# Routing 18 of 24 token tiles inside attention, a shorter chain for the last six, and gates from a second set of products

## The chip, the cores and the metric

One of the eight cores of a Trainium2 chip runs the program. The metric is the device time of one execution in microseconds (us). Its engines are TensorE (PE, with its weight loads as PEld), VectorE (DVE), ScalarE (ACT), GpSimd (POOL) and SyncE (SP), which here only issues DMAs.

## What is computed

```
q, k, v: (4, 8, 768, 64)       # attention with 4 sink keys and a window of 128
scores = where(is_sink | in_window, scale * q @ k.T, -1e9)
a = softmax(scores);  x = (a @ v) as rows: (3072, 512)

logits = x @ w_gate + modality_bias[modality_id]          # 8 experts
e = argmax(logits);   gate = softmax(logits)[e]
y[rows of e] = gate * (relu(x[rows of e] @ w1[e]) @ w2[e])   # w1: 512x1024

h = y @ w_in;  out = (h * sigmoid(1.702 h)) @ w_out       # w_in: 512x2048
```

## The kernel before

Attention runs over 4 batches of 48 steps each (8 heads, 6 query tiles of 128 rows, `each_step`). In step n PE multiplies the scores of tile n (`scores`), turns the probabilities of tile n - 3 (`turn_probs`, copied out of PSUM by ACT, and by DVE for the last tile of a head: `move_probs`) and weighs the values of tile n - 4 (`weigh_values`). DVE masks each tile (`mask_scores`), and every sixth step it scales a finished head (`finish_head`), which also gives that head's share of the router logits. Heads go out to `x_rows` in DRAM in pairs (`store_pair`). GpSimd only splits q and k of coming heads into a high and a low part (`split_qk`); it is through with the last head at 206.6 us.

Each product of large matrices is three products of such high and low parts (`fp32r`).

Behind attention comes the routing, for all 24 tiles of 128 tokens at once. DVE adds the biases, takes the maximum, makes a one-hot of the chosen expert (ties go to the lowest number), and the gate from `exp` on ACT. PE multiplies the one-hot with a triangle and with ones (L738, L739), DVE sums the tile counts by doubling (L1244), and so knows each token's place among the tokens of its expert. From counts it makes `table` (which expert each of 32 slots of 128 rows belongs to, where a run of one expert begins, how many there are), signals `runs_ready`, and SP loads the first expert's weights in four quarters of 1 MB (`load_run`). DVE then makes masks: `oh_val` (tile of the slot times token number, gate high, gate low) and `oh_slot` (row in the slot). The inverse, which token stands in which row of which slot, is the sum of 24 products of these (L744). From it come `gather_i`, `scatter_i` and `gates`.

The experts run slot by slot: POOL gathers the 128 rows (`gather`), PE turns them (`turn_xs`), ACT and DVE split them (`xs_high`, `xs_low`), PE multiplies up (`up`), turns h (`turn_h`), multiplies down (`down`), DVE scales by the gate and POOL scatters. For slot 0 `up` needs the first split and the high and low parts of w1 (`w_highs` on ACT, `w_lows` on DVE). The loads of the next expert (`load_run` in a loop) wait until the low parts of the same quarter are made. This data uses 3 experts in 26 slots. Then the dense layers follow.

Every order is written by hand: each engine executes its list in order, and semaphores are all that connects them. The helper `then` makes an engine wait for its own last instruction.

## Time and profile before

| what | value |
| --- | --- |
| median of 3 runs (lowest to highest) | 1146.12 us (1145.73 to 1149.06) |
| the profiled execution | 1148.82 us |
| its span in the profile | 1146.6 us |
| PE busy | 1103.9 us, 96% |
| DVE, ACT, POOL busy | 37%, 33%, 26% |
| chain that ended last | PE 92%, DVE 4% |
| attention | 0 to 231 us |
| routing, until the first expert product | 231 to 272 us |
| experts, then dense layers | 272 us to the end |

Busy time is that of instructions on the engine. In a timeline a row starts with its start and its length in us; at its end, in brackets, stands how long the engine had been idle and who ended that. Matmuls are pipelined, so their lengths overlap, and distances of starts say more. `PEclk` is the granted clock of PE, 1.00 at 2.4 GHz and 0.50 at 1.2 GHz.

### The profile page before, as it was taken

To read this page: it belongs to the slowest core of one execution; us is meant where nothing else is said; L and a number is where in the kernel's file an instruction comes from. 1 tells how busy PE (TensorE), PEld (TensorE's weight loads), DVE (VectorE), ACT (ScalarE), POOL (GpSimd) and SP (SyncE) were. 2 spreads that over 40 slices of the span, in tenths; PEclk is the share of its full clock that TensorE was granted. 3 is DMA by queue.
4 is the path that set the end of the run, shared out by engine and by line. 5 is a ranking of instruction groups with operands and counts; after the bars stand their busy time and mean duration, and the time that the engine had idled before them with its cause. 6 is when DMAs were issued, how large, how long until landed. Compare 5 with 4: busy or idle time off the path is not lost.

```text
span 1146.6 us, 18452 instructions
## 1 busy us (share of the span) xinstructions
PE 1103.9 (96%) x5844; PEld 933.2 (81%) x5845; DVE 429.7 (37%) x1109; ACT 376.8 (33%) x780; POOL 299.9 (26%) x394
## 2 busy tenths in 40 slices
PE   9999999926999999999999999999999999999998
PEld 9999999915888888888887888888888888888887
DVE  5666656685222224222265223323223222222222
ACT  3666666613222233212254222222222222222222
POOL 8888889202662212212110001001001001000100
PEclk9999999956999999999999999999999999999999
DMA  9999998136111115211133001101000100000000
GB/s 221 229 247 238 234 239 224 47 102 242 37 37 55 37 46 192 67 53 46 37 107 123 19 1 46 27 0 46 18 9 37 27 9 19 18 0 0 37 1 37
DMA packets 57390, 92.01 MB, mean 80 GB/s; under 512 B 7936, under 2 KB 32768, under 8 KB 57344
## 3 DMA queue, kind: packets, MB, share of 16 engines
q1 hardware_dynamic: 51584, 72.56, 23.7%
q0 software_dynamic: 5760, 18.89, 4.8%
q8 instruction: 23, 0.38, 0.2%
q14 instruction: 23, 0.19, 0.1%
HBM read 72.02 MB, written 19.41 MB: 80 GB/s over the span
## 4 chain that ended last, share of the span: by engine, by line
PE 92%; DVE 4%; issue 1%; ACT 1%; POOL 1%; DVEq 0%; ACTq 0%; POOLq 0%
PE psum L837 8%; PE psum L828 8%; PE psum L830 8%; PE psum L839 8%; PE psum L829 8%; PE psum L838 8%; PE psum L686 6%; PE psum L770 4%; PE psum L771 4%; PE psum L772 4%; PE psum L795 4%; PE psum L797 4%; PE psum L796 4%; PE psum L661 3%; PE psum L649 2%; PE psum L782 2%
## 5 line engine op out<-in xcount | busy, mean ns | idle before, releaser
L1421 DVE TENSOR_TENSOR g<-psum,g 128x512 f32<-128x512 f32 x96 | 66.3, 691 | 306.5 <-ACT g L1024 306.4
L1024 ACT ACTIVATE g<-psum 128x512 f32<-128x512 f32 x96 | 57.5, 599 | 319.0 <-PE psum L830 316.1
L828 PE MATMUL psum<-x2T,win_hi 128*128 (+1 forms) x384 | 153.1, 399 | 2.3 <-DVE g L1421 2.3
L837 PE MATMUL psum<-w_hi,gT_hi 128*128 128x512 f32 x384 | 153.2, 399 | 0.0
L830 PE MATMUL psum<-x2T,win_lo 128*128 (+1 forms) x384 | 152.5, 397 | 0.0
L829 PE MATMUL psum<-x2T,win_hi 128*128 (+1 forms) x384 | 152.0, 396 | 0.0
L839 PE MATMUL psum<-w_hi,gT_lo 128*128 128x512 f32 x384 | 150.4, 392 | 0.0
L838 PE MATMUL psum<-w_lo,gT_hi 128*128 128x512 f32 x384 | 149.3, 389 | 0.0
L618 POOL DMA_INDIRECT out<-o_out,out_rows x20 | 19.5, 976 | 424.3 <-ACT o_out L1037 419.7
L686 PE MATMUL psum<-v_sb,pT 128*128 128x73 f32 x704 | 106.0, 269 | 1.7
L1148 DVE CUSTOM_DVE_ANT_0 s_msk<-psum,mask_sb 128x260 f32<-128x260 f32 (+1 forms) x192 | 74.8, 403 | 74.1 <-PE psum L650 38.9
L686 PEld LDWEIGHTS psum<-v_sb,pT 128*128 128x128 f32 x704 | 93.4, 191 | 8.2 <-DVE pT L1160 6.7
L908 ACT ACTIVATE probs<-s_msk,negmax 128x260 f32<-128x260 f32 (+1 forms) x192 | 93.4, 495 | 12.3 <-DVE negmax L1148 12.3
L1424 DVE TENSOR_TENSOR gT_lo<-g,gT_hi 128x512 fp32r<-128x512 f32 x96 | 66.5, 693 | 65.9 <-ACT gT_hi L1028 65.9
L770 PE MATMUL psum<-w_hi,xsT_hi 128*128 128x512 f32 x208 | 84.5, 406 | 4.1 <-DVE xsT_lo L1375 4.1
L828 PEld LDWEIGHTS psum<-x2T,win_hi 128*128 128x128 f32 x384 | 72.5, 189 | 19.2 <-issue 2.7
L830 PEld LDWEIGHTS psum<-x2T,win_lo 128*128 128x128 f32 x384 | 72.4, 189 | 18.1
L829 PEld LDWEIGHTS psum<-x2T,win_hi 128*128 128x128 f32 x384 | 72.4, 188 | 17.1
L839 PEld LDWEIGHTS psum<-w_hi,gT_lo 128*128 128x128 f32 x384 | 72.0, 188 | 17.2
L838 PEld LDWEIGHTS psum<-w_lo,gT_hi 128*128 128x128 f32 x384 | 72.2, 188 | 15.7
L1028 ACT CAST gT_hi<-g 128x512 fp32r<-128x512 f32 x96 | 59.6, 620 | 75.7 <-DVE g L1421 75.7
L837 PEld LDWEIGHTS psum<-w_hi,gT_hi 128*128 128x128 f32 x384 | 72.1, 188 | 14.8
(200 smaller groups left out, 1950.7 us busy)
## 6 DMA issues: line engine op xcount, KB each, us to landing
qk_raw<-qkT SPq DMA_DIRECT2D x64, 384.0 KB, 9.2
stage<-w SPq DMA_DIRECT2D x12, 1024.0 KB, 6.1
x<-y_rows SPq DMA_DIRECT2D x24, 256.5 KB, 2.6
vT_sb<-vT SPq DMA_DIRECT2D x16, 384.0 KB, 10.4
v_sb<-vP SPq DMA_DIRECT2D x16, 384.0 KB
x_rows<-x_sb SPq DMA_DIRECT2D x16, 384.0 KB, 8.0
win_raw<-w_in SPq DMA_DIRECT2D x16, 256.0 KB, 10.3
stage<-w_out SPq DMA_DIRECT2D x4, 1024.0 KB, 6.5
```

The costliest lines, as they stand in the source:

```text
L686: mm = pe.matmul(o, pT[:, n % 2, k * P:(k + 1) * P], v_sb[:, c, kb, half * VEXT:(half + 1) * VEXT], start=(i == 0 and k == 0), stop=(k == ...
L770: pe.matmul(psum[:, HB[hf], :], xsT_hi[:, c, :], hi, start=(c == 0), stop=False)
L828: pe.matmul(bank, wh, hi, start=(c == 0), stop=False)
L829: pe.matmul(bank, wh, lo, start=False, stop=False)
L830: mm = pe.matmul(bank, win_lo[:, c, f * P:(f + 1) * P], hi, start=False, stop=(c == CH - 1))
L837: pe.matmul(psum[:, OB[t], :], gh, hi, start=(f == 0), stop=False)
L838: pe.matmul(psum[:, OB[t], :], gh, lo, start=False, stop=False)
L839: return pe.matmul(psum[:, OB[t], :], gT_lo[:, f % 4, t * P:(t + 1) * P], hi, start=False, stop=(f == F2C - 1))
L908: act.activation(probs[:, n % RING, 0:width[i]], s_msk[:, n % RING, 0:width[i]], ACT.Exp, bias=negmax[:, n % 8:n % 8 + 1], scale=-1.0).the ...
L1148: dve.tensor_tensor_reduce(s_msk[:, n % RING, 0:width[i]], psum[:, S_ps[n % 3], 0:width[i]], mask_sb[:, min(i, MASKS - 1), 0:width[i]], -S ...
L1421: dve.tensor_tensor(g32[:, f % 2, :], psum[:, FB[f % 2], :], g32[:, f % 2, :], ALU.mult)\
L1424: dve.tensor_tensor(gT_lo[:, f % 4, :], g32[:, f % 2, :], gT_hi[:, f % 4, :].bitcast(F32), ALU.subtract).then_inc(gT_split, 1)
```

## The change

Bias, maximum, one-hot, exponential and gate of the first 18 tiles (batches 0 to 2) move into steps 29 to 43 of the last batch, on DVE, with the exponential on ACT at step 39. POOL adds up their one-hots tile by tile (`seen`), PE multiplies their ranks at step 41 (`rank_early`), and POOL makes their `oh_slot`. For the six tiles of the last batch seven heads are summed at step 49, and behind the last head DVE has a short list (`add_last_head` to `choose`). Their ranks come from eight small products, with counts over all tiles among them, so the sum by doubling is gone. `x_sb` of the last head is scaled only behind the one-hot.

The first expert's number is computed ahead of the tables and has a semaphore of its own, `expert_known`; SP loads its w1 then, its w2 once the first gather has landed, and reads the table later. The inverse is multiplied for the token numbers alone; `gather_i` comes from it in one operation, and the gates come from a second set of 24 products. The tables (`make_tables`, `make_spare`) move behind the second low part of w1 on DVE, and the end of the scatter table goes to POOL, between its second and third gather. Between these products PE gets dummy products of the identity: 16, 40, 12 and 8 (`keep_going`).

```diff
@@ SP
+            sp.wait_ge(expert_known, 1)
+            load_run(0, sp.value_load(first_e[0:1, 0:1], min_val=0, max_val=E - 1))
+            load_win(B * PAIRS - 1)
             sp.wait_ge(runs_ready, 1)
...
-            load_run(0, sp.value_load(table[0:1, RUN_E:RUN_E + 1], min_val=0, max_val=E - 1))
@@ SP, load_run, quarter q of run 0
+                        if q == 2:
+                            sp.wait_ge(gathered, 16)
@@ POOL
+            pool.wait_ge(onehot_ready, 1)
+            for t in range(PRE):
+                then(pool.tensor_tensor(seen[:, t + 1, :], seen[:, t, :].bitcast(F32), onehot[:, t, :].bitcast(F32),
+                                        ALU.add))
+            pool.sem_inc(tiles_seen, 1)
+
+            pool.wait_ge(rows_known, 1)
+            for t in range(PRE):
+                pool.tensor_scalar(oh_slot[:, t, :], iota_row[:], rank_p[:, t:t + 1], None, ALU.is_equal)\
+                    .then_inc(rows_marked, 1)
+
+            def finish_scatter():
...
+                pool.wait_ge(spare_known, 1)
+                then(pool.tensor_tensor(t1, iota_slot[:], t1, ALU.subtract))
...
+                then(pool.tensor_scalar(scatter_i[:, 0:SLOTS], t1, iota_dump[:, 0:1], None, ALU.add))
...
+            gather(0)
+            gather(1)
+            finish_scatter()
+            gather(2)
+            pool.wait_ge(runs_ready, 1)
             total = pool.value_load(table[0:1, TOTAL:TOTAL + 1], min_val=NTILE - 4, max_val=SLOTS - 4) + 4
-            for t in range(3):
-                gather(t)
-            pool.wait_ge(tables_ready, 2)
@@ PE
+            def rank_early():
+
+                pe.wait_ge(onehot_ready, 1)
+                pe.wait_ge(tiles_seen, 1)
...
+                pe.matmul(at, tri[:], onehot[:, 0:PRE, :].rearrange("p t e -> p (t e)"), start=True, stop=False)
+                pe.matmul(at, ones[:], seen[:, 0:PRE, :].rearrange("p t e -> p (t e)"), start=False, stop=True)\
+                    .then_inc(ranks_ready, 1)
...
+            def keep_going(times):
+                for _ in range(times):
+                    pe.matmul(psum[:, XB, 0:P], ident[:], ident[:], start=True, stop=True)
+
+            pe.wait_ge(scores_masked, B * HT + AHEAD)
+            keep_going(16)
+
+            pe.wait_ge(onehot_ready, 2)
...
+            mm.then_inc(ranks_ready, 1)
+            keep_going(40)
+
+            pe.wait_ge(rows_marked, PRE)
             for t in range(NTILE):
-                if t % GT == 0:
-                    pe.wait_ge(ohs_ready, t // GT + 1)
-                mm = pe.matmul(psum[:, 2, 0:3 * SLOTS], oh_slot[:, t, :], oh_val[:, t].rearrange("p a s -> p (a s)"),
+                if t in (0, PRE):
+                    pe.wait_ge(ohs_ready, 1 + t // PRE)
+                mm = pe.matmul(psum[:, 2, 0:SLOTS], oh_slot[:, t, :], tile_tok[:, t, :],
                                start=(t == 0), stop=(t == NTILE - 1))
...
+            keep_going(12)
+
+            pe.wait_ge(heads_done, B * H + AHEAD)
+            pe.wait_ge(gates_marked, 1)
+            for t in range(NTILE):
+                mm = pe.matmul(psum[:, O_ps[1], 0:2 * SLOTS], oh_slot[:, t, :],
+                               tile_gate[:, t].rearrange("p a s -> p (a s)"), start=(t == 0), stop=(t == NTILE - 1))
+            mm.then_inc(gates_ready, 1)
+            keep_going(8)
...
+            turn_xs(0)
+            up(0, 0)
+            turn_xs(1)
+            pe.wait_ge(runs_ready, 1)
@@ ACT
+            first_high(0, w1_high)
             xs_high(0)
+            first_high(1, w1_high)
+            first_high(2, w2_high)
+            first_high(3, w2_high)
             relu(0)
             xs_high(1)
@@ DVE, the last batch
+            def route_early(n):
+
+                if n == 29:
+                    then(dve.tensor_scalar(from_end[:], iota_row[:, 0:E], -1.0, float(E), ALU.mult, ALU.add))
+                    pick_bias(0)
+                if n == 30:
+                    for m in range(1, NM):
+                        pick_bias(m)
+                if n == 31:
+                    add_biases(pre)
+                    find_best(pre)
+                if n == 33:
+                    find_lead(pre)
+                if n == 35:
+                    then(dve.tensor_scalar(seen[:, 0, :], from_end[:], 0.0, None, ALU.mult))
+                    choose(pre)
...
+                if n == 41:
+                    make_gates(pre, 1)
+                if n == 42:
+                    take_ranks(pre, psum[:, VW_ps, 0:PRE * E].rearrange("p (t e) -> p t e", e=E), 1)
...
@@ DVE, behind attention
+            add_last_head()
+            find_best(own)
+            find_lead(own)
+            choose(own)
...
+            dve.tensor_scalar(first_e[:], e_cnt[:, 1, 0:1], -1.0, float(E), ALU.mult, ALU.add).then_inc(expert_known, 1)
...
+            first_low(0, w1_high, w1_split)
             xs_low(0)
+            first_low(1, w1_high, w1_split)
+            make_slot_gates()
+            make_tables()
+            make_spare()
...
+            first_low(2, w2_high, w2_split)
             xs_low(1)
+            first_low(3, w2_high, w2_split)
```

Three places show how the lists stand. PE first, from attention's last product to the first product of an expert; `ident` alone is a dummy, `ident,xs` turns the first slot's rows, `w_hi,xsT_hi` is the expert's. Before:

```order
L691 MATMUL psum<-v_sinks,pT_sinks 128x4x73
L738 MATMUL psum<-onehot,tri 128x192
L739 MATMUL psum<-onehot,ones 128x192
L744 MATMUL psum<-oh_val,oh_slot 128x96 x24
L800 TENSOR_LOAD table
L800 ISA x2
L755 MATMUL psum<-ident,xs 128x128 x4
```

PE in the changed kernel, from the 16 dummies on (seven more small products of one-hots stand between the ranks' first and the 40):

```order
L825 MATMUL psum<-onehot,ones 128x16
L825 MATMUL psum<-onehot,ones 128x8
L809 MATMUL psum<-ident 128x128 x40
L835 MATMUL psum<-tile_tok,oh_slot 128x32 x24
L809 MATMUL psum<-ident 128x128 x12
L843 MATMUL psum<-tile_gate,oh_slot 128x64 x24
L809 MATMUL psum<-ident 128x128 x8
L854 MATMUL psum<-ident,xs 128x128 x4
```

Two sets of products and 76 dummies now stand ahead of the first rows, and the read of the table is gone from there.

DVE in steps 30 to 32 of the last batch; `s_msk` is a tile's mask, `pT` the copy that PE waits for. Before:

```order
L1148 ISA s_msk,negmax<-psum,mask_sb 128x128
L1148 ISA negmax 128x1
L1148 ISA s_msk,negmax<-psum,mask_sb 128x260
L1148 ISA negmax 128x1
L1148 ISA s_msk,negmax<-psum,mask_sb 128x260
L1148 ISA negmax 128x1
L1159 COPY pT_sinks<-psum 128x128
L1160 COPY pT<-psum 128x256
```

DVE there in the changed kernel (four more operations, up to `bias_of`, stand ahead of the first row's mask, in step 29):

```order
L1245 TENSOR_SCALAR mod_eq<-mod_f 128x24
L1247 TENSOR_TENSOR biases<-mod_eq,bias_sb 128x192
L1249 TENSOR_TENSOR bias_of<-bias_of,biases 128x192
L1354 ISA s_msk,negmax<-psum,mask_sb 128x260
L1354 ISA negmax 128x1
L1259 TENSOR_TENSOR lg<-lg,bias_of 128x144
L1268 TENSOR_REDUCE best<-lg 128x18
L1354 ISA s_msk,negmax<-psum,mask_sb 128x260
L1354 ISA negmax 128x1
L1365 COPY pT_sinks<-psum 128x128
L1366 COPY pT<-psum 128x256
```

Nine operations now stand between the masks ahead of the copy.

POOL from the last split of q and k to the third gather; brackets name what a row waits for. Before:

```order
L549 TENSOR_TENSOR q_st<-qk_raw,q_st 64x768 [waits qk_rounded]
L552 TENSOR_TENSOR k_lo<-qk_raw,k_hi 128x6x128 [waits qk_split]
L554 TENSOR_TENSOR k_lo<-qk_raw,k_hi 128x6x4
L592 TENSOR_LOAD table [waits x_stored3,x_stored2,tables_ready,x_stored1,x_stored0]
L592 ISA x2
L574 COPY gather_col<-gather_i 128x1
L578 DMA xs<-x_rows,gather_col 128x512 [waits gather_set,xs_turned]
```

POOL in the changed kernel, where seven more rows of the same kind stand between the two on `tokens` and the last:

```order
L591 TENSOR_TENSOR seen<-seen,onehot 128x8 [waits onehot_ready]
L591 TENSOR_TENSOR seen<-seen,onehot 128x8 [waits pool_step] x17
L597 TENSOR_SCALAR oh_slot<-iota_row,rank_p 128x128 [waits pool_step,rows_known]
L597 TENSOR_SCALAR oh_slot<-iota_row,rank_p 128x128 x17
L635 DMA xs<-x_rows,gather_i 128x512 [waits tables_ready,x_stored3,xs_turned,x_stored2,x_stored0,x_stored1]
L635 DMA xs<-x_rows,gather_i 128x512 [waits xs_turned]
L604 TENSOR_TENSOR tokens<-iota_slot,tokens 128x32 [waits spare_known]
L605 TENSOR_TENSOR tokens<-tokens 128x32 [waits pool_step]
```

The first gather stands without a table read or copy ahead of it, the third behind nine operations.

## Rows read from the trace of the kernel before

**Rows 1.** Windows: stretch, length, busy PE, PEld, DVE, ACT, POOL, clock, DMA, GB/s.

```profile
231.00:272.00 41.00, 8.41 (x33) 7.37 (x34) 34.06 (x100) 10.04 (x8) 5.26 (x4) 0.53 0.41 138
```

**Rows 2.** Timeline behind attention's last product, DVE.

```profile
231.03 0.17 DVE L1165 TENSOR_SCALAR rden<-psum 128x6 f32<-128x6 f32 x1 [1.30 <-PE psum L691]
231.23 0.19 DVE L1167 RECIPROCAL rden<-rden 128x6 f32<-128x6 f32 x1
```

**Rows 3.** Timeline from the table to the inverse products, all engines.

```profile
247.13 0.20 DVE L1287 CAST table<-table_f 128x75 int32<-128x75 f32 x1
...
250.48 25.98 SPq L428 DMA_DIRECT2D stage<-w  x8
250.49 0.96 DVE L1310 TENSOR_TENSOR tile_eq<-iota_row,pos_t 128x768 f32<-128x768 f32 x1
...
255.20 5.36 PE L744 MATMUL psum<-oh_val,oh_slot 128*128 128x96 f32 x24 [17.82 <-DVE oh_slot L1316]
255.63 1.90 ACT L965 CAST w_hi<-stage 128x2048 fp32r<-128x2048 f32 x1 [5.96 <-DMA stage<-w]
```

**Rows 4.** Timeline from the first gather to the first expert product, all engines.

```profile
263.55 1.15 POOL L578 DMA_INDIRECT xs<-x_rows,gather_col  x1 [0.96 <-POOL gather_col L574]
...
266.37 4.49 DVE L1360 TENSOR_TENSOR w_lo<-stage,w_hi 128x2048 fp32r<-128x2048 f32 x2 [0.95 <-DVE gates L1346]
...
267.12 1.12 PE L755 MATMUL psum<-ident,xs 128*128 128x128 f32 x4 [6.57 <-DMA xs<-x_rows,gather_col]
...
268.28 0.59 ACT L981 CAST xsT_hi<-psum 128x512 fp32r<-128x512 f32 x1 [2.66 <-PE psum L755]
...
271.71 0.77 PE L770 MATMUL psum<-w_hi,xsT_hi 128*128 128x512 f32 x1 [3.48 <-DVE xsT_lo L1375]
```

**Rows 5.** Timelines of SP, POOL, DVE and PE, second gather to first down projection.

```profile
268.89 7.57 SPq L428 DMA_DIRECT2D stage<-w  x4
...
269.54 2.17 POOL L578 DMA_INDIRECT xs<-x_rows,gather_col  x1 [0.83 <-POOL gather_col L574]
276.63 0.18 POOL L574 COPY gather_col<-gather_i 128x1 int32<-128x1 int32 x1 [4.92 <-DMA xs<-x_rows,gather_col]
...
281.47 0.69 DVE L1375 TENSOR_TENSOR xsT_lo<-psum,xsT_hi 128x512 fp32r<-128x512 f32 x1 [5.61 <-ACT xsT_hi L981]
...
287.99 0.60 PE L755 MATMUL psum<-ident,xs 128*128 128x128 f32 x4
288.34 0.48 PE L795 MATMUL psum<-w_hi,hT_hi 128*128 128x512 f32 x1
```

**Rows 6.** Windows where the clock falls and where it rises again (PEclk is third last).

```profile
233.60:233.80 0.20, 0.00 (x0) 0.00 (x0) 0.17 (x2) 0.00 (x0) 0.00 (x0) 0.50 0.95 289
...
277.00:278.00 1.00, 1.00 (x4) 0.81 (x3) 0.00 (x0) 0.60 (x1) 0.00 (x0) 0.54 1.06 391
```

**Rows 7.** Windows of L728, the identity products at the start (PE, PEld, PEclk, DMA, GB/s).

```profile
13.30:14.25 0.95, 0.89 (x8) 0.92 (x8) 1.00 0.97 207
```

**Rows 8.** Timelines of DVE and PE, steps 31 to 36 of the last batch.

```profile
209.03 0.43 DVE L1148 CUSTOM_DVE_ANT_0 s_msk<-psum,mask_sb 128x260 f32<-128x260 f32 x1 [0.50 <-ACT probs L908]
...
209.94 0.43 DVE L1148 CUSTOM_DVE_ANT_0 s_msk<-psum,mask_sb 128x260 f32<-128x260 f32 x1 [0.47 <-PE psum L650]
...
210.29 0.29 DVE L1159 COPY pT_sinks<-psum 128x128 f32<-128x128 f32 x1
...
210.96 0.67 PE L686 MATMUL psum<-v_sb,pT 128*128 128x73 f32 x4
...
214.97 0.36 DVE L1137 TENSOR_TENSOR bias_of<-c,bias_sb 128x192 f32<-128x192 f32 x1
```

**Rows 9.** POOL: timeline of two dependent operations, then one line's durations.

```profile
6.20 0.29 POOL L500 TENSOR_SCALAR_AFFINE_SELECT mask_sb<-mask_sb 128x128 f32<-128x128 f32 x1
6.63 0.29 POOL L502 TENSOR_SCALAR_AFFINE_SELECT mask_sb<-mask_sb 128x128 f32<-128x128 f32 x1
...
L554 POOL TENSOR_TENSOR k_lo<-qk_raw,k_hi x31: 218/228/237, 16.0 to 206.3; 128x24 fp32r<-128x24 f32 x31
```

More of the change, by code:

```diff
@@ L221, in program @@
         e_cnt = place("e_cnt", [P, 6, E])
-        tokens = place("tokens", [P, 3, SLOTS])
+        tokens = place("tokens", [P, 4, SLOTS])
         table_f = place("table_f", [P, TAB])
@@ L943, in step, with gate_exps @@
                     spread_sinks(b, n // (2 * QT))
-            each_step(step)
-            act.wait_ge(shifted, 1)
-            act.activation(r_b, r_a, ACT.Exp).then_inc(exped, 1)
-            act.wait_ge(runs_ready, 1)
-            for c in range(PAIRS):
-                act.wait_ge(x_stored[c], DMA * B + DMA)
-            last = act.value_load(table[0:1, TOTAL:TOTAL + 1], min_val=NTILE - 4, max_val=SLOTS - 4) + 2
+                if b == B - 1 and n == EXP_AT:
+                    gate_exps(slice(0, PRE), 1)
+            def gate_exps(tiles, part):
+                act.wait_ge(shifted, part)
+                act.activation(exps_of[:, tiles, :], below[:, tiles, :], ACT.Exp).then_inc(exped, 1)
+            each_step(step)
+            gate_exps(slice(PRE, NTILE), 2)
             def run_and_first(t):
@@ new lines, in _, with col, row, shape_of @@
+            e_col = iota_row[:, 0:E].rearrange("p (s o) -> p s o", o=1).broadcast_to(sq)
+            e_row = iota_row[:, 0:E].rearrange("p (o e) -> p o e", o=1).broadcast_to(sq)
+            full, pre, own = [P, NTILE, E], slice(0, PRE), slice(PRE, NTILE)
+            def col(v, shape):
+                return v.rearrange("p (t o) -> p t o", o=1).broadcast_to(shape)
+            def row(v, shape):
+                return v.rearrange("p (o e) -> p o e", o=1).broadcast_to(shape)
+            def shape_of(tiles):
+                return [P, tiles.stop - tiles.start, E]
@@ new lines, in _ @@
+            busy, runs_before = e_cnt[:, 4, :], e_cnt[:, 5, :]
+            then(dve.tensor_tensor(tend, base_e[:], tiles, ALU.add))
+            then(dve.tensor_scalar(busy, tiles, 0.0, None, ALU.is_gt))
+            tab = [P, SLOTS, E]
+            ends, counted = (e_tab[:, k].rearrange("p (s e) -> p s e", e=E) for k in range(2))
+            slot_col = col(iota_row[:, 0:SLOTS], tab)
+            then(dve.tensor_tensor(ends, slot_col, e_cnt[:, 3:4, :].broadcast_to(tab), ALU.is_ge))
+            then(dve.tensor_tensor(counted, ends, e_cnt[:, 4:5, :].broadcast_to(tab), ALU.mult))
```

427 lines of the change are left out of this document (242 added, 185 removed).

## The prediction

> **What bounds the kernel now.** I read the windows first, then the timeline from 226 to 300 us, then the timelines of DVE, PE and POOL inside the last batch. PE is busy almost everywhere except between the two halves of the program: from 231 to 272 us it works 8.4 of 41 us and its clock is down to 0.53 on average [rows 1]. Attention's last product is done at 231.0 (DVE, which waited for it, starts at 231.03 [rows 2]); the first expert matmul starts at 271.71 [rows 4]. In between one thing at a time happens: DVE computes logits, one-hots and ranks, all tables, four wide masks; PE multiplies 24 tiles; then the row indices, the gather, a transpose, a split. From 288.34 on, where the first down projection starts [rows 5], PE has no wait that the change reaches, so I carry the change from 231.0 to that point: what it wins there is the gain. The profiled execution took 1148.82 us with a span of 1146.6, so 2.2 us lie outside it, and the median of the runs is 1146.12. I take the gain off the median.
>
> **Step 1, routing inside attention (a loss).** DVE gets bias, maximum and one-hot work of the first 18 tiles in steps 29 to 36 of the last batch. A narrow DVE operation costs 0.20 us start to start [rows 2], one of 192 columns 0.40 (0.36 and the hand-over) [rows 8], so one of 144 some 0.31. Step 29: three narrow and one wide, 1.0. Step 30: one narrow, two wide, 1.0. Step 31: two of 144, 0.6. That is 2.6 us ahead of the copy of the turned probabilities of step 29, in a stretch where DVE idles 0.50 and 0.47 [rows 8]. PE takes that copy at once: copies start at 210.29, last 0.6, and the product that reads them starts at 210.96 [rows 8]. So PE loses 2.6 - 1.0 = **1.6 us**. The biases that this replaces stood at step 36, with slack behind them; there the new work (about 1.6 us) only takes their place. At steps 41 to 43 DVE gets 2.0 us more, but PE's own delay (next) covers it.
>
> The one-hot of the early tiles is then ready near 216.6 (before's step 35 mask, plus 1.6, plus 0.5 of its own). POOL adds it up in 18 dependent additions of 8 columns. The nearest rows are a dependent pair of POOL operations, 0.43 us start to start, and its 24-column addition of 0.23 [rows 9]: bounds 0.28 and 0.43 each. I take 0.35, nearer to the small one plus the hand-over (0.14 between the rows of the pair). 18 x 0.35 = 6.3, so 222.9, and PE stands before its early rank product at 222.0: **0.9 us** (0 to 2.4), and 0.2 for the two products. Attention ends 2.7 us later, at 233.7; the bounds are 1.0 and 4.5. All times below are without this 2.7, which is taken off at the end.
>
> **Step 2, from attention to the row indices.** The last batch's chain on DVE is now eight operations of at most 48 columns behind the last product (0.20 to 0.24 each), 231.03 to about 233.1. But PE's queue has 16 dummy matmuls ahead of the rank products. A dummy is two records; 8 records take 0.89 us at full clock [rows 7], 0.22 a dummy, so 16 are 3.6: ranks start at 234.5, not 233.1. The 8 rank products go at the rate of small products, 24 in 5.36 us at half clock [rows 3], 0.11 each at full clock: 0.9, done 235.5. Then 40 dummies: 8.9, to **244.4**. DVE in that time needs six narrow operations (first expert, 236.8), two, two of 64 columns, two of 192, one narrow (238.7), the wide comparison of 768 columns at 0.96 [rows 3], the tokens (1.0), and its six tiles' rows (0.96 and a narrow one): 242.0. So it isn't DVE that is late, it is the dummies, by 2.4 us. 24 inverse products: 2.6, to 247.0. Row indices in one operation: 247.3.
>
> **Step 3, to the first expert matmul.** The gather goes straight from those indices; POOL started 0.96 us after its copy and PE had the rows 3.57 us later [rows 4], so rows are there at 251.8. That is cover, not path: PE first does 12 dummies (2.7, hidden behind DVE) and waits for the gates' masks. DVE: four narrow operations, two of 768 columns: 0.9 + 2.0, ready 250.2. 24 gate products 2.6, 8 dummies 1.8, transposes 0.60 [rows 5]: 255.2. ACT's high part 0.59 [rows 4] and DVE's low part 0.69 [rows 5], with hand-overs 1.4: **256.6**, against 271.71. Weights do not decide it: expert known at 236.8, SP issues within 1 to 3 us, the first quarter arrives 5.1 us after issue and is cast in 1.90 [rows 3], its low part takes 2.25 [rows 4]; all that ends by 252.5.
>
> **Step 4, from there to the first down projection.** ACT casts the second quarter only behind the first rows: 255.9 + 1.9 = 257.8, DVE's low part 2.25: 260.1. An up projection took 5.8 at full clock, start included (24 matmuls from the split at 281.47 + 0.69 to 287.99 [rows 5]); half of one is 2.8, so PE waits 0.7 and ends the second half at 262.9. Behind the low part DVE has slot gates (0.4), tables (15 operations, 3.4: 263.9), spare counts (1.3: 265.2), a low part (2.25) and only then the second tile's split (0.7): 268.2. The second up projection therefore starts at 268.2 and ends at 273.8; that is a wait of 2.3 us that the kernel before hasn't got.
> POOL finishes the scatter table before its third gather: spare counts at 265.2, nine operations of about 0.37: 268.5, gather starts 269.3. Alone a gather lands after 3.6. But SP has the table at 263.9, reads four registers (3.1 us from the table, 247.13 + 0.20, to the first issue at 250.48 in the kernel before [rows 3]) and issues the next expert's weights from 267 on. The gather that started at 269.54 under such loads (SP issued from 268.89 on) was back at 276.63, 7.1 us [rows 5]. With three quarters queued at 2.7 each behind the 5.1 (267.0 + 5.1 + 5.4 = 277.5) I take 8: 277.3. PE waits 3.5, transposes, starts down at **277.7**. Before: 288.34. Gain 10.6, less 2.7 of step 1: **7.9 us**. Part of it is the clock: the kernel before ran the first 6.1 us at half rate (0.50 from 233.6, up in the slice 277 to 278 [rows 6]), 3.0 us lost, which the dummies are to save.
>
> **Rivals.**
> *The third gather isn't held up.* It lands 3.6 us after it starts, at 272.9, before PE wants it: 3.5 us more, a gain of 11.4, **1134.7**. For it: the transfer is small, and how many quarters are queued at that moment depends on SP's register reads. Against it: the 7.1 us of a gather behind fresh loads [rows 5]. Chance 0.20. The Trainium skill, DMA: Bandwidth & Descriptors, section Queues, rings and completion order, says that a DMA engine takes turns between the queues that have work, packet by packet; by that rule the gather would pass the weights and the sum would be this rival's. The trace does not agree well: under loads a gather took twice its time alone.
> *The clock falls in the new waits.* PE is idle 2.3 and 3.5 us in step 4; in the kernel before it was down by 233.6, 2.6 us after the last work [rows 6]. If it falls once where nothing hides it, the price is that of the kernel before: 3.0 us. Gain 4.9, **1141.2**. Chance 0.15; against it, PE has worked densely up to the wait.
> *POOL's additions are slow.* If each costs what POOL shows between a copy and its dependent DMA, 0.83 [rows 5], 18 take 14.9 and PE stands 9.5 us instead of 0.9: gain -0.7, **1146.8**. It eats the gain from 0.8 us an addition on. Chance 0.05.
> *Slower: the dummies run at half clock.* If the half rate (1.2 GHz) has set in before the first block of them, each dummy costs 0.44, and the small products double. The first two blocks, ranks and inverse products then take 16.0 us more; the third block, 5.3, outlasts DVE's masks by 2.2; gate products, last block and transposes take 4.9 more: 23.0 in all. The gain turns into a loss of 15.2: **1161.3**. It eats the gain from some 36 half-rate dummies on, fewer if the products fall with them. Against it: the clock reads 1.00 over the stretch of the same dummies at the start [rows 7], and PE has no gap before them. Chance 0.05.
> *It does less than it says:* the dummies may cover what was won, as step 2 has it for 2.4 us; that is in the forecast.
>
> **How the numbers follow.** Forecast 0.53 at 1146.1 - 7.9 = **1138.2**, its own range 1135 to 1141 (step 1: +1.7, -1.8; POOL and register reads 1 us each). Gather early 0.20 (1132.5 to 1136.5), clock 0.15, slow additions 0.05, slow dummies 0.05, something smaller than 3.4 us for other reasons 0.02. The range from 1132.5 to 1142.5 leaves out the last three and the tails. A measurement of this kernel can tell about 0.3%, 3.4 us, from no change. Faster by more: nearly all of 0.53 and 0.20 and most of the clock's 0.15: 0.86. Within: the rest of these and the slow additions, 0.08. Slower: 0.06.
>
> **What would show it.** In the profile of the changed kernel: PE waiting at the copy of step 29 by 1.6 us and before the early rank product by about 1; its clock at 1.00 from 231 on; the inverse products starting right behind the 40 dummies and not behind a DVE wait; the first expert matmul 12 us earlier than 271.71; waits of PE on the second split (2.3) and on the third gather (3.5), with weights in flight. It is wrong if the third gather lands in under 5 us, if the early additions take above 8 us in all, or if PE waits for the inverse masks instead of running dummies.

## The result, and the profile after

The changed kernel takes 1150.32 us (median of 19 runs, 1147.94 to 1158.09), the kernel before 1146.72 beside it (19 runs, 1145.73 to 1149.06): ratio 1.0035, 95% interval [1.002, 1.005]. It is slower by 0.35%, and outside the predicted range. The profiled execution took 1149.0 us with a span of 1147.1, so it is one of the shorter ones, 0.2 us above the profiled one of before (0.5 in the spans); the medians are 3.6 us apart. The 19 executions of before lie in two groups, 1145.7 to 1146.7 and 1148.1 to 1149.1 us, and the profiled one is of the upper group. The two traces explain 0.5 us; the other 3.1 are differences between executions of one kernel that they do not show.

| stretch (us) | before | forecast | after |
| --- | --- | --- | --- |
| attention's end | 231.03 | +2.7 | 238.22 (+7.2) |
| from there to the first expert product | 40.7 | 25.6 | 26.65 |
| from there to the first down projection | 16.6 | 21.1 | 24.0 |
| first down projection starts at | 288.34 | 280.4 | 288.86 |

From there to the end it is 858.3 us before and 858.2 after. So in these traces the routing chain did get shorter by 14 us, and all of it was given back: 7.2 in attention, 7.4 between the first expert product and the first down projection.

The equal ends hide two falls of PE's clock that cancel. In both kernels PE waits 2.28 us for `g` ahead of the first product of the dense layers. Up to that product the changed kernel loses 1.5 us (318.1 us from the first down projection, 316.6 before), all of it at half clock behind 288.86. Behind it the traced execution of before loses 1.5 us, since its clock falls there and that of the changed kernel does not: the same products take 0.63 and 0.40 us. Rows of PE, before and then after:

```profile
604.93 0.49 PE L828 MATMUL psum<-x2T,win_hi 128*128 x1 [2.28 <-DVE g L1421]
...
606.24 0.63 PE L829 MATMUL psum<-x2T,win_hi 128*128 x1
```

```profile
606.96 0.49 PE L928 MATMUL psum<-x2T,win_hi 128*128 x1 [2.28 <-DVE g L1610]
...
607.74 0.40 PE L928 MATMUL psum<-x2T,win_hi 128*128 x1
```

PE's timeline after, the rows at which the forecast has a term (start, length, at the end in brackets the idle time before and who ended it). `pT` is the copy of the turned tiles 29 and 41, `tile_tok` the inverse products, `tile_gate` the gate products, `ident` alone dummies, `ident,xs` the turning of rows, `w_hi,xsT_hi` up projections, `w_hi,hT_hi` the first down projection:

```profile
215.18 0.67 PE L745 MATMUL psum<-v_sb,pT 128*128 128x73 f32 x4 [2.36 <-DVE pT L1366]
...
230.15 0.67 PE L745 MATMUL psum<-v_sb,pT 128*128 128x73 f32 x4 [1.41 <-DVE pT L1366]
...
251.34 2.83 PE L835 MATMUL psum<-tile_tok,oh_slot 128*128 128x32 f32 x24
254.01 4.55 PE L809 MATMUL psum<-ident 128*128 128x128 f32 x24
258.32 2.85 PE L843 MATMUL psum<-tile_gate,oh_slot 128*128 128x64 f32 x24
...
264.87 0.50 PE L869 MATMUL psum<-w_hi,xsT_hi 128*128 128x512 f32 x1 [1.40 <-DVE xsT_lo L1550]
268.28 0.50 PE L869 MATMUL psum<-w_hi,xsT_hi 128*128 128x512 f32 x1 [0.39 <-DVE w_lo L1570]
276.42 0.79 PE L869 MATMUL psum<-w_hi,xsT_hi 128*128 128x512 f32 x1 [2.13 <-DVE xsT_lo L1550]
287.89 0.66 PE L854 MATMUL psum<-ident,xs 128*128 128x128 f32 x4 [3.12 <-DMA xs<-x_rows,gather_i]
288.86 0.79 PE L894 MATMUL psum<-w_hi,hT_hi 128*128 128x512 f32 x1 [0.31 <-issue]
```

Windows after (columns as in [rows 1]; the clock is third last). The first answers [rows 1]: PE is busy 25.3 of 26.7 us where it was busy 8.4 of 41. The others are where the clock is down:

```profile
238.20:264.90 26.70, 25.30 (x213) 25.06 (x212) 15.70 (x46) 5.02 (x6) 3.77 (x5) 0.94 0.45 148
...
230.00:232.00 2.00, 1.85 (x9) 1.55 (x10) 0.44 (x3) 0.11 (x1) 2.00 (x4) 0.71 0.04 8
232.00:234.00 2.00, 2.00 (x11) 2.00 (x11) 1.49 (x7) 0.85 (x3) 2.00 (x5) 0.50 0.00 0
...
254.00:256.00 2.00, 2.00 (x14) 2.00 (x14) 1.59 (x6) 0.00 (x0) 0.39 (x1) 0.68 0.00 0
256.00:258.00 2.00, 2.00 (x12) 2.00 (x10) 2.00 (x3) 0.00 (x0) 1.28 (x1) 0.50 0.05 8
...
277.00:281.00 4.00, 4.00 (x11) 3.12 (x10) 2.58 (x3) 0.00 (x0) 3.35 (x7) 0.50 1.05 401
...
290.00:292.00 2.00, 2.00 (x6) 1.53 (x5) 0.00 (x0) 0.00 (x0) 1.99 (x2) 0.50 0.46 127
```

The mean clock rose from 0.979 to 0.993. What a low clock costs on the path changed less. Before, the half rate fell into 41 us in which PE had little to do; it cost 3.0 us in the first expert products and 1.5 at 605, and it doubled the 24 inverse products (5.36 us for 2.67), for which DVE stood 2.44 us (before):

```profile
260.59 0.19 DVE L1323 TENSOR_SCALAR tokens<-psum 128x32 f32<-128x32 f32 x1 [2.44 <-PE psum L744]
```

In the changed kernel it comes four times up to 293 us, each time under work, where the forecast had it at full rate. A window of 2 us at 0.50 loses 1.0. It loses 1.7 us at 230 to 235, of which 1.35 reach the end of attention; 1.6 in the dummies at 254 (24 records take 4.3 us, 2.7 at full clock), of which 1.1 are on the path, since the gate masks come late too; 2.6 in the second up projection (hidden, since the third gather is awaited anyway); 1.6 behind 288.86. That is some 4.1 us on the path.

DVE after, steps 29 to 32, ahead of PE's row at 215.18. It answers [rows 8]; the first column is the start:

```profile
210.94 0.36 DVE L1247 TENSOR_TENSOR bias_of<-mod_eq,bias_sb 128x192 f32<-128x192 f32 x1
211.53 0.29 DVE L1354 CUSTOM_DVE_ANT_0 s_msk<-psum,mask_sb 128x128 f32<-128x128 f32 x1 [0.23 <-DVE bias_of L1247]
...
213.62 0.30 DVE L1268 TENSOR_REDUCE best<-lg 128x18 f32<-128x144 f32 x1
214.15 0.43 DVE L1354 CUSTOM_DVE_ANT_0 s_msk<-psum,mask_sb 128x260 f32<-128x260 f32 x1 [0.23 <-DVE best L1268]
...
214.71 0.41 DVE L1366 COPY pT<-psum 128x256 f32<-128x256 f32 x1
```

Each group of routing work costs 0.23 us more than its operations: `then` waits for the last of them before the mask may start.

GpSimd and DVE after, where the scatter table is finished ahead of the third gather, and the line of the 18 additions:

```profile
273.30 2.28 DVE L1570 TENSOR_TENSOR w_lo<-stage,w_hi 128x2048 fp32r<-128x2048 f32 x1
273.47 2.22 POOL L604 TENSOR_TENSOR tokens<-iota_slot,tokens 128x32 f32<-128x32 f32 x1 [8.25 <-DVE tokens L1518]
...
275.50 0.68 DVE L1550 TENSOR_TENSOR xsT_lo<-psum,xsT_hi 128x512 fp32r<-128x512 f32 x1
275.77 0.25 POOL L605 TENSOR_TENSOR tokens<-tokens 128x32 f32<-128x32 f32 x1
276.10 2.28 DVE L1570 TENSOR_TENSOR w_lo<-stage,w_hi 128x2048 fp32r<-128x2048 f32 x1
276.12 2.42 POOL L606 TENSOR_SCALAR tokens<-tokens 128x32 f32<-128x32 f32 x1
...
219.23 5.12 POOL L591 TENSOR_TENSOR seen<-seen,onehot 128x8 fp32r<-128x8 f32 x18 [11.74 <-DVE onehot L1279]
```

The same kind of operation on 32 columns takes 0.25 us beside DVE's `xsT_lo`, which reads one operand from PSUM, and 2.2 to 2.4 when it meets a low part of w, which reads both from SBUF, the on-chip memory; it then ends 0.1 to 0.2 us behind that.

### The profile page after: what moved, and what is told of

It reads as the page before. It is cut to its first block, busy times and chain, and to the rows that moved or that the text cites. A ratio compares the mean times of both kernels' runs of the same rounds, so it can differ in the third digit from the quotient of the medians.

```text
span 1147.1 us, 18894 instructions
## 1 busy us (share of the span) xinstructions
PE 1124.4 (98%) x6026; PEld 953.5 (83%) x6027; DVE 426.7 (37%) x1100; ACT 378.5 (33%) x781; POOL 321.0 (28%) x436
## 4 chain that ended last, share of the span: by engine, by line
PE 90%; DVE 3%; issue 2%; ACT 2%; POOL 1%; DMA 1%; ACTq 0%; DVEq 0%; POOLq 0%
PE psum L937 8%; PE psum L928 8%; PE psum L939 8%; PE psum L930 8%; PE psum L929 8%; PE psum L938 8%; PE psum L745 5%; PE psum L894 4%; PE psum L896 4%; PE psum L895 4%; PE psum L871 4%; PE psum L870 4%; PE psum L869 4%; PE psum L720 2%; PE psum L881 2%
## 5 line engine op out<-in xcount | busy, mean ns | idle before, releaser
L894 PE MATMUL psum<-w_hi,hT_hi 128*128 128x512 f32 x208 | 84.5, 406 | 0.5 <-issue 0.3
```

The lines of the kernel that those rows point to most:

```text
L894: pe.matmul(psum[:, YB, :], hT_hi[:, f, :], hi, start=(f == 0), stop=False)
```

## The experiments

All are compared with the kernel before, run beside them on the same chip; its median there was 1148.26 (a1 to a4), 1146.85 (b1 to b4), 1148.44 (c1 to c3, a5) and 1146.76 (d1), its lowest and highest values within 0.6 us of those above. Its median still moves by 1.7 us, so differences of medians between these sets of runs are good to about 1.7 us. Each kernel of the table ran 4 to 11 times.

| kernel | median us | ratio to before, 95% interval |
| --- | --- | --- |
| a1_head_waits | 1150.34 | 1.0014 [1.0003, 1.0025] |
| a2_spread | 1149.69 | 1.0018 [1.0007, 1.0029] |
| a3_dummies | 1144.46 | 0.9960 [0.9945, 0.9976] |
| a4_order | 1143.32 | 0.9957 [0.9942, 0.9971] |
| b1_slots | 1152.89 | 1.0046 [1.0024, 1.0068] |
| b2_combo | 1137.70 | 0.9924 [0.9908, 0.9941] |
| b3_best | 1142.81 | 0.9952 [0.9927, 0.9976] |
| b4_late | 1151.57 | 1.0031 [1.0015, 1.0047] |
| c1_free | 1144.60 | 0.9976 [0.9965, 0.9987] |
| c2_all | 1133.83 | 0.9884 [0.9867, 0.9902] |
| c3_no_dummies | 1143.73 | 0.9964 [0.9947, 0.9981] |
| a5_gather_first | 1143.75 | 0.9974 [0.9962, 0.9985] |
| d1_tuned | 1128.94 | 0.9838 [0.9824, 0.9852] |

**What attention lost: own waits, or the work?** The first run takes only waits away: behind a head's logits DVE does not wait for itself.

```diff
@@ finish_head, add_heads (a1_head_waits)
-                then(part)
+                if b == B - 1 and h == H - 1: then(part)
+                else: steps[0] += 1; part.then_inc(dve_step, 1)
+                dve.wait_ge(dve_step, steps[0])        # ahead of the sum over heads
```

> The changed kernel, with DVE no longer waiting for its own last instruction behind each head's logits and behind the sum over heads of batches 0 to 2. In the changed kernel's trace the first mask behind that sum is 0.22 us late, and PE is later by 0.43 to 0.47 us at step 9 of every batch, 1.8 us in all by step 28 of the last batch. Theory A (the added waits are the cause): scores of step 28 of the last batch start at 205.7 to 206.1 us instead of 207.64, the span shrinks by 1.5 to 1.9 us. Theory B (the shift comes from somewhere else, such as the fetch of a longer instruction list): it stays within 0.4 us of 207.64.

The start of the scores of step 28 of the last batch, against before (205.68), is +1.96 in the changed kernel and +0.7 here: the waits cost 1.3 us, less than theory A's 1.5 to 1.9 and far more than theory B's 0.4. The median does not show it (1150.34 for 1150.32, from two sets of runs). But the rest shows what a wait of PE can trigger. Row of PE and window of a1_head_waits:

```profile
213.87 1.13 PE L745 MATMUL psum<-v_sb,pT 128*128 128x73 f32 x4 [2.34 <-DVE pT L1370]
```

```profile
214.00:230.00 16.00, 16.00 (x71) 15.40 (x72) 6.45 (x33) 4.71 (x14) 3.67 (x18) 0.50 0.00 0
```

The same wait of 2.3 us at the copy of tile 29 as in the changed kernel, and behind it 16 us of attention at half clock, with PE busy all along. This execution took 1156.67 us; the changed kernel has three of its length (1158), which were not traced. So this wait costs 2.2 us in one trace and 10 in another.

The second run keeps that edit and moves the early routing:

```diff
@@ route_early (a2_spread): steps
-  29, 30, 31, 33, 35, 36, 37, 41, 42, 43
+  1, 9, 13, 21, 25, 33, 45, and the gates of the early tiles behind attention
```

> As the run before it, and the early tiles' routing is cut into pieces that stand where DVE idled 1.1 us or more in the kernel before (steps 1, 9, 13, 21, 25, 33, 45 of the last batch) instead of steps 29 to 43; the early gates' sum goes behind the last head. Theory A (DVE's queue ahead of the copies of steps 29 and 41 is what holds PE up, and the clock falls in the waits it makes): attention ends at 231 to 232 us instead of 238.0, PE has no wait above 0.6 us in the last batch, its clock stays at 1.00 there, and the span shrinks by 6 to 7 us. Theory B (added work on DVE costs wherever it stands, since DVE is near its limit): half of it at most, attention ends at 234 or later.

Attention still loses 6.1 us up to step 47, in waits of 1.7 at step 4 and again at 16, with half clock behind the second: theory B. This spoke for a price of the work wherever it stands. I then took its place in the cycle of six steps for the cause (DVE makes the last copy of a head in steps 6k + 2, and PE takes it at once), and put the work right behind that copy:

```diff
@@ route_early (b1_slots, with the edit of a1): steps
-  29, 30, 31, 33, 35, 36, 37, 41, 42, 43
+  6, 9, 12, 18, 21, 24, 42, 45
```

> The early routing stands elsewhere in the last batch: its first part at steps 6 and 9, the rest at 12, 18, 21, 24, 42 and 45, that is only where a head's last copy has just been made (6k + 3) or the next is two steps away (6k); the waits of VectorE for its own last instruction behind each head are gone too. Nothing behind attention changes. Theory A (place in the cycle): the work costs only where it stands one to three steps ahead of the copy that PE takes at once; here at most 1.5 us of the 7.2 that attention lost is left, no wait of PE there is over 1 us, the clock stays at 1.00 through attention, the median falls to some 1145. Theory B (the work costs wherever it stands): as with the spread over steps 1 to 45, attention loses 5 to 6 us and the median is 1149 to 1151.

That theory fell as it stood: 1152.89, a wait of PE of 3.5 us at step 10, attention 11 us longer. The cause is in the rows of DVE and of GpSimd (both b1_slots):

```profile
182.90 1.62 DVE L1321 TENSOR_SCALAR from_end<-iota_row 128x8 f32<-128x8 f32 x1
184.56 0.18 DVE L1244 CAST mod_f<-mod_i 128x24 f32<-128x24 int32 x1
184.77 1.66 DVE L1245 TENSOR_SCALAR mod_eq<-mod_f 128x24 f32<-128x24 f32 x1
186.46 0.36 DVE L1247 TENSOR_TENSOR bias_of<-mod_eq,bias_sb 128x192 f32<-128x192 f32 x1
```

```profile
182.68 1.82 POOL L578 TENSOR_TENSOR q_st<-qk_raw,q_st 64x768 fp32r<-64x768 f32 x1
184.57 1.82 POOL L581 TENSOR_TENSOR k_lo<-qk_raw,k_hi 128x768 fp32r<-128x768 f32 x1
```

An operation on 8 columns takes 1.62 us, since GpSimd's subtraction had started 0.22 us before it: it ends 0.02 us behind that. The next narrow one ends 0.04 us behind the second subtraction. The rows of DVE ahead of the two waits of a2_spread show the same, so its loss does not speak for a price of the work wherever it stands. They end 0.03 to 0.17 us behind subtractions of GpSimd that had started at 175.27, 177.16 and 192.52 (1.81, 1.83 and 1.82 us long):

```profile
175.67 1.44 DVE L1321 TENSOR_SCALAR from_end<-iota_row 128x8 f32<-128x8 f32 x1
...
177.36 1.67 DVE L1324 TENSOR_SCALAR mod_eq<-mod_f 128x24 f32<-128x24 f32 x1
...
192.69 1.82 DVE L1263 TENSOR_TENSOR lg<-lg,bias_of 128x144 f32<-128x144 f32 x1
```

In the changed kernel, where GpSimd is idle from 207.5 on, the same two took 0.17 and 0.18. The Trainium skill, SBUF — State Buffer, section Who interferes with whom, says it: VectorE in a two-port mode shares one pair of ports with GpSimd, and whoever issues first keeps it for the whole instruction while the other stands still; with two inputs from SBUF, VectorE gets in the way of GpSimd's reads. These rows agree, and those of GpSimd at 273.47 above are the same in the other direction.

So both conditions together:

```diff
@@ route_early (c1_free, with the edit of a1): steps
-  29, 30, 31, 33, 35, 36, 37, 41, 42, 43, PE's early ranks at 41
+  30 (biases), 33 (maximum), 36 (one-hot), 42 (gates), 45 (ranks), PE's at 43
```

> The same operations of the early routing as in b1_slots and in the same places of the six-step cycle, but only after GpSimd's last split of q and k: biases at step 30, maximum at 33, one-hot at 36, gates at 42, ranks at 45 (PE's early ranks at 43). In b1_slots operations of 8 and of 24 columns took 1.62 and 1.66 us while GpSimd's subtraction of two operands from memory ran (182.68 to 186.4), and the wait of PE was 3.5 us. Theory A (place in the cycle, and GpSimd idle, both needed): every such operation takes 0.2 to 0.4 us, no wait of PE in attention is over 0.8 us, attention loses at most 2 us of the 7.2, clock 1.00 throughout, median 1144 to 1146. Theory B (2 us of VectorE's work in a head cost about 2 us wherever they stand): attention loses 4 us or more, waits of 1.4 to 2.4 us stay, median 1148 or more.

As theory A had it, in the main: 1144.60. Every operation of the early routing takes 0.17 to 0.36 us. Attention loses 2.5 us (theory A allowed 2), 1.3 of it in one wait of 1.45 us (allowed 0.8) and 1.0 ahead of the last batch, and the clock reads 1.00 up to 248. The median is 5.7 under the changed kernel's with nothing changed behind attention.

**What the dummies cost, and what they give.**

```diff
@@ PE (a3_dummies)
-            keep_going(16) / (40) / (12) / (8)
+            keep_going(10) / (22) / (12) / none
```

> The changed kernel with 10, 22, 12 and 0 dummy products in place of 16, 40, 12 and 8; attention as in the changed kernel. In its trace the ranks start 1.2 us after their one-hot, the inverse products 2.5 us after the last mask and 4 us after the first 18 could start, and 8 dummies stand ahead of the first transpose. Theory A (the dummies lie on the path): the first expert product comes 26.65 - 6.5 = about 20 us behind attention's last product, the span shrinks by 5 to 7 us if the next waits stay as long. Theory B (the dummies pay for themselves, since without them the clock falls): the clock reads 0.5 somewhere between the ranks and the first expert product, the small products double, and the gain is under 2 us.

From attention's end to the first expert product it is 19.65 us for 26.65, and the median falls by 5.9, theory A: the dummies outlasted DVE, as step 2 had it. The clock fell to half from 257 to 262 all the same. Leaving all dummies out, on top of the next edits:

> b2_combo (1137.7) without any dummy product. Theory A (the dummies pay by the clock): it falls to 0.50 within 3 us of attention's end; inverse products take 5.3 for 2.8, gate products 5.3 for 2.8, ranks and transposes 1.3 more, the first up projection starts at half rate and loses some 3: 9 us in all, 1146 to 1147. Theory B (VectorE's chain sets the time, PE has slack): products at half rate are hidden in part, 1140 to 1142. Theory C (the dummies only stand in the way): 1137 or less.

Rows of PE of c3_no_dummies:

```profile
253.89 5.27 PE L833 MATMUL psum<-tile_tok,oh_slot 128*128 128x32 f32 x24 [5.07 <-DVE tile_tok L1451]
...
262.22 5.30 PE L840 MATMUL psum<-tile_gate,oh_slot 128*128 128x64 f32 x24 [3.06 <-DVE tile_gate L1483]
```

6.0 us more than b2_combo, between theories A and B: both sets of products double (5.3 for 2.8), and DVE hides part of it. From attention's end to the first down projection it is 43.1 us for 38.5, so 4.6 are the dummies' own; in the profiled execution attention ran at half clock from 215 to 231 as well, which b2_combo's did not. Some dummies pay, and 44 serve better than 76; whether fewer would do is not tested.

**The order behind the first expert product.**

```diff
@@ POOL and DVE (a4_order; a5_gather_first has the first two lines only)
-            finish_scatter(); gather(2)
+            gather(2); finish_scatter()
-            make_tables(); make_spare(); first_low(2); xs_low(1); first_low(3)
+            make_tables(); xs_low(1); first_low(2); first_low(3); make_spare()
```

> The changed kernel with two changes of order: POOL starts the third gather ahead of the end of the scatter table, and DVE splits the second tile's rows ahead of the low part of w2 and of the spare counts. Theory A (those orders make the waits, and the waits let the clock fall): the wait for the second tile's split (2.1 us) and the wait for the third gather (3.1 us) go, the clock is at 1.00 over the second up projection and the first down projection, and the first down projection starts 6 to 8 us earlier behind the first up projection (24.0 us in the changed kernel, 16.5 to 18 here); span down by 6 to 8 us. Theory B (the third gather is slow because of the weights in flight, whenever it starts): the wait for it only shrinks to about 2 us, the gain is 3 to 4 us.

> The changed kernel with one edit: the third gather is issued ahead of the scatter table on GpSimd; VectorE's order is left (the second rows' low part comes behind the first low part of w2). Theory A (the two halves of a4_order are of two separate waits): PE's wait of 3.1 us for the third rows goes, and with it a second fall of the clock (2 us), the wait for the second low part (2.1 us) and its half clock stay: 1145 to 1147 against 1150.3. Theory B (the gather was waited for only because all else was late): without the other edit nothing is gained, 1149 to 1151.

a4_order: first down projection 17.0 us behind the first expert product for 24.0, median 7.0 lower. Its third gather starts at 273.21 instead of 281.69:

```profile
273.21 0.94 POOL L635 DMA_INDIRECT xs<-x_rows,gather_i  x1 [7.33 <-PE psum L854]
```

PE does not wait for those rows at all: theory A. a5_gather_first gives nearly all of it (1143.75), more than either theory expected: its wait of 2.2 us for the second split stays, and the clock with it, but the wait for the gather and the fall behind it (288.86 to 292.2 in the changed kernel) are gone. By the medians, from two sets of runs, the order on DVE is then worth 0.4 us, too little to tell from nothing. By the traces the first down projection comes 43.6 us behind attention's end in a4_order and 46.7 in a5_gather_first, with half clock in the second up projection of the latter alone. What that order is worth stays open.

> Fewer dummy products (10, 22, 12, 0 for 16, 40, 12, 8) and the new order (third gather ahead of the scatter table; the second rows' low part ahead of the low parts of w2; spare counts last) together, attention left as in the changed kernel. Theory A (the two pay in different waits): gains add up, 5.9 + 7.0 under 1150.3, so 1137.4; first expert product 20 to 21 us behind attention's end and the first down projection 17 us behind that. Theory B (the earlier start runs into the same weights): the transfers of the second quarters and the table's reads set the end, so the first down projection starts where it did with the order alone, 282.5, and the median is 1142 to 1144.

1137.70 (4 runs), within 0.3 of the sum of the two gains: theory A. The first expert product comes 19.8 us behind attention's end and the first down projection 18.7 behind that, for the 17 of the expectation: PE waits 2.3 us for the low part of h.

**All together, and is it worth routing early at all?**

> All three: the routing behind the copies as in the run b1_slots, fewer dummies, the new order. If all costs are separate, the median is that of b2_combo less the 5 us that b1_slots should win: 1132. If the routing's cost in attention is unavoidable, it equals b2_combo within 1 us. If an earlier end of attention only meets the same arrival of weights, it lies between, the first expert product waiting for a low part of w1.

1142.81, slower than b2_combo, which none of the three cases had. It carries b1_slots' places, and with them a wait of 3.5 us and half clock in attention. With c1_free's places instead:

> c1_free with the fewer dummies (10, 22, 12, 0) and the new order of b2_combo (1137.7). Theory A: the same 5 us come off, 1132 to 1133. Theory B: as c1_free shows nothing, neither does this: 1136 to 1138. If the loads of weights set the first expert product once attention ends earlier, it lies between and a wait for a low part of w1 shows.

1133.83 (4 runs); 3.9 us under b2_combo, not the full 5, and no wait for a low part of w1 shows. In the traces attention ends 4.5 us earlier, and from there to the first down projection it is 38.5 us in both.

> The new order, and no routing inside attention: only the biases stand in step 36, as in the kernel before, and three constants in 42. Maximum, one-hot, POOL's 18 additions, exponential and ranks of the first 18 tiles stand behind attention's last product, with 34, 30 and 12 dummies to keep PE busy. Theory A (early routing costs more in attention than it spares behind it): attention ends at 231 to 232 instead of 238.2, the chain behind it grows by 2.2 (operations) + 5.1 (additions) + 1.5 (ranks), about 9, less 4 of the dummies that no longer stand ahead of it: the median is within 2 us of b2_combo, 1136 to 1140. Theory B (early routing pays): the 18 row masks on POOL (10.4 us behind the ranks) hold the inverse up as well, it comes 6 us or more later than in b2_combo against attention's end at 231 and the median is above 1141.

Theory B. Attention ends at 233.2 instead of 238.3, but the 18 masks on GpSimd take 12.2 us (243.4 to 255.6) and PE stands for them (PE, b4_late), then runs at half clock until 264 and again from 268 to 276:

```profile
255.63 5.30 PE L834 MATMUL psum<-tile_tok,oh_slot 128*128 128x32 f32 x24 [5.35 <-POOL oh_slot L597]
```

The first down projection starts 12.6 us later than in b2_combo. Routing early pays; it has to stand where it fits.

**The last run** moves work by the room that the rows show: 1.0 to 1.2 us behind a head's last copy, 2 us at step 36, where the kernel before had its biases.

```diff
@@ DVE (d1_tuned, on c2_all)
   n == 30: from_end, seen[0], pick_bias(0)
   n == 33: pick_bias(1)
   n == 36: add_biases, find_best, find_lead, choose, shift
   n == 39: tri, ones
@@
-            make_tables(); xs_low(1); first_low(2); first_low(3); make_spare()
+            make_tables(); make_spare(); xs_low(1); first_low(2); first_low(3)
```

> c2_all (1133.8) with two things moved. In attention: the bias work is split over steps 30 and 33 (1.2 and 1.0 us), maximum, one-hot and shift stand together in step 36, where the kernel before had 2 us of biases at no cost, the two constants in 39. c2_all lost 1.3 us at step 34, behind 1.8 us of biases in step 30. Behind attention: the spare counts stand directly behind the tables again, where VectorE idled 2.86 us for the second rows' split; in c2_all they stood behind the low parts of w2, and PE waited 2.3 us for the low part of h. Theory A (a place is worth its room: 1.2 us behind a copy, 2 us at every twelfth step): attention loses at most 1.2 us instead of 2.5, PE's wait for the low part of h falls to about 1.1, median 1131 to 1132.5. Theory B (the 1.3 us at step 34 are the price of having the work at all, and the wait for h is set by the low parts of w2): 1133.5 to 1134.5.

1128.94 (5 runs), 2 us better than theory A. It is 1.6% faster than the kernel before (0.9838 [0.9824, 0.9852]) and beats both. The largest waits of PE in d1_tuned from 172 to 300 us (line, total, times, longest), then those of the changed kernel in the same stretch:

```profile
PE psum L868 <- DVE xsT_lo L1553: 2.1, 2, 1.4
PE psum L745 <- DVE pT L1365: 0.6, 2, 0.5
PE psum L880 <- ACT h L1085: 0.6, 1, 0.6
```

```profile
PE psum L745 <- DVE pT L1366: 4.0, 3, 2.4
PE psum L869 <- DVE xsT_lo L1550: 3.5, 2, 2.1
PE psum L854 <- DMA xs<-x_rows,gather_i: 3.1, 1, 3.1
PE psum L881 <- issue: 1.5, 1, 1.5
```

In d1_tuned attention loses 1.65 us up to step 47 (theory A: 1.2), of which 1.05 stand ahead of the last batch, so the work inside it costs 0.6. The wait for the low part of h is gone (theory A: 1.1 left), and the first down projection starts without a wait, 16.3 us behind the first expert product and 19.4 us before that of the kernel before:

```profile
268.98 0.48 PE L893 MATMUL psum<-w_hi,hT_hi 128*128 128x512 f32 x1
```

## Why the prediction was wrong, by its own steps

By its steps the forecast was -7.9 us and the traces show +0.5: step 1 took 4.5 us more than forecast, step 3 1.05 and step 4 2.9. The medians lie 3.1 us further apart, which no step covers: the forecast had one time for each kernel, and executions of one kernel differ (the changed kernel's mean clock runs from 0.985 to 0.994).

**Step 1** is the step that failed: 7.2 us for 2.7, and above its own upper bound of 4.5. Its parts:
- The waits of DVE for itself behind each head's logits and behind the sum over heads were in the diff and not priced at all. They cost 1.3 of the +1.96 us up to step 28; 0.42 of the rest is in batch 0 and in every variant, 0.2 is there at the first score, and I did not find their cause.
- Steps 29 to 31: 2.24 for 1.6. The operations took what was forecast (2.6 us); the difference is the hand-over to the mask, three times 0.23 us, which the sum had as nothing.
- Steps 41 to 43: "PE's own delay covers it" is false. A delay of PE moves the product and the copy together; it makes no room between them. 1.44 us; c1_free, with the same operations at steps 42 and 45, loses nothing there.
- The additions of GpSimd were taken too dear (5.12 for 6.3) and the wait for them did not come, since all else was late: the 0.9 priced for it was 0, which hides part of the other misses. 0.2 for the products was right.
- Behind the second wait the clock fell: 0.75 up to step 47 and 0.6 behind it. The rival on the clock named step 4 alone, and had not thought of attention.

**Step 2** held: ranks 3.5 us behind the first dummy (3.6), 40 dummies in 8.9 us, 24 inverse products in 2.7, and the dummies late by 2.5 us against DVE's rows (ready at 248.81), as forecast (2.4). a3_dummies confirmed it with more than that: the first expert product comes 7.0 us earlier, since the 6 of the first block and the last 8 stood in the way too (14 of 0.22 us, 3.1); the 1.4 left over are not traced to a cause.

**Step 3:** 26.65 for 25.6. The one miss is the third block of dummies, at half clock without any gap in PE's work before it. In a2_spread, with the same list of PE behind attention, the clock stays at 1.00 there, and the stretch takes 25.54. All later links (gates to transposes to split, 6.55 for 6.4) held.

**Step 4:** second half 3.4 us behind the first (3.5), the second up projection 11.55 behind it (11.6), wait 2.13 (2.3). Then the third gather: the nine operations of GpSimd took 7.4 us for 3.3, because two met DVE's low parts. [rows 5] had shown it: the gather's own row of 2.17 us (0.97 for the next one) stands beside such a low part, and I gave all 7.1 us of that gather to the loads. The third gather started 16.8 us behind the first expert product (12.7), landed 6.2 us after its start (8) and PE waited 3.12 (3.5). The first down projection is 2.9 us later than forecast.

**The rivals.** *The clock falls in the new waits*, 0.15, is what came, and more often than priced: it had one fall of 3.0 us, the trace shows four, some 4.1 us on the path. It was no rival to the rest but came on top of it. *The third gather isn't held up* did not come: 6.2 us under loads for 3.6 alone. By the turn-taking between queues of the Trainium skill, DMA: Bandwidth & Descriptors, section Queues, rings and completion order, it should have passed the loads; this landing does not show that. a5_gather_first, whose third gather starts ahead of the next expert's loads, has the first down projection 3.9 us nearer to the first expert product (20.1 for 24.0), close to the rival's price of 3.5. *Additions slow* and *dummies at half clock* did not come in the form given. The slower side was given 0.06 and had to come from one mechanism; what came was the sum of several misses of the same sign. That the first down projection ends what the change reaches was wrong as well: 1.5 us at half clock stand behind it, and only a fall at 605 in the traced execution of before makes up for them.

Not settled: why the same wait of 2.3 us for the copy of tile 29 is followed by 16 us at half clock in some executions and by none in others, and what the fall at 254, with PE busy since 238, answers to.

## What to carry to other kernels

Work that is moved beside a pipelined loop costs nothing only where its duration with the hand-over fits between two copies that the bottleneck takes at once, and while no other engine holds the ports it needs: list that room step by step, from the trace, before choosing the step. A late bottleneck engine gives no such room. Price a wait of PE by what its clock may do behind it, not by its length, and let dummies end with the work they cover.

## What the runs showed of the hardware

- VectorE and GpSimd stop one another for the whole instruction: 8 columns in 1.62 us for 0.17 (b1_slots), 32 columns in 2.22 for 0.25 (the changed kernel). VectorE's `xsT_lo`, with one operand from PSUM, did not hold up such an operation (0.25).
- A wait of PE of 2.3 us in attention was followed by 16 us at 0.50 under full work in a1_head_waits, by none at that place in the changed kernel. A wait of 2.28 us at 605 was followed by some 3 us at 0.50 in the traced execution of before, by none in that of the changed kernel.
- PE's clock fell to 0.50 at 255 in the changed kernel with PE busy without a gap from 238 on (window 238 to 252 at 1.00), on dummies and small products. In c1_free it fell likewise, with PE busy before it and 0.50 from 250 to 252; in a2_spread, on the same list of PE, it did not fall up to 274.
- A mask behind an operation that DVE waits for itself starts 0.23 us after its end.
